# Attention, mixture of experts and a second feed-forward in one kernel: GpSimd work between scatters, other iterations for the first weights, the last attention iteration reordered

## The reference

```python
# 1. attention, B=4, H=8, S=576, D=64, causal window of 64
scores = where(0 <= row - col < 64, (q @ k.T) / sqrt(D), -1e9)
x = (softmax(scores) @ v)                 # -> [2304, 512]
# 2. mixture of 8 experts, two of them per token
noisy = x @ w_gate + log1p(exp(x @ w_noise)) * noise
top2, top2_w = the two largest of noisy, softmax of the two
out[token] += top2_w * (relu(x[token] @ w1[e]) @ w2[e])      # F = 1024
# 3. feed-forward
h = out @ w_in;  y = (h * clip(h + 3, 0, 6) / 6) @ w_out      # F2 = 2048
```

## Time and profile before

| | before |
|---|---|
| median of 3 runs | 1040.16 us (1039.94 to 1040.4) |
| profiled execution | 1048.24 us, its span 1046.5 us |
| PE busy / PEld busy | 96% / 85% of the span |
| DVE / ACT / POOL busy | 40% / 22% / 40% |
| first matmul of expert 0 (L1502) | starts at 158.16 us |
| PE busy before 160 us / after | 132.5 of 160 us / 876.5 of 886.5 us |

### The profile page before, as it was taken

One profiled execution on the slowest core, in us unless ns is written; L12 is line 12 of the kernel. 1 busy time (PEld: TensorE's weight loads), 2 busy tenths in 40 slices (PEclk: granted clock), 3 DMA queues, 4 the chain that ended last, 5 costly groups with the idle time before them and its releaser, 6 DMA issues.

```text
span 1046.5 us, 19876 instructions
## 1 busy us (share of the span) xinstructions
PE 1009.0 (96%) x8098; PEld 892.9 (85%) x8098; DVE 414.5 (40%) x879; ACT 234.0 (22%) x537; POOL 417.9 (40%) x276
## 2 busy tenths in 40 slices
PE   6899879999999999999999998999999999999998
PEld 5777658898999898999989987899999999999997
DVE  3466644322223122222222147644545445354433
ACT  4655531111111121111111112121111121111211
POOL 3555543898391918466482937400101001000000
PEclk9989879999999999999999999999999999999999
DMA  9877575867162625436251444110101001100000
GB/s 201 182 195 197 167 231 183 250 207 231 61 202 72 199 93 156 156 101 211 80 156 58 133 129 161 41 45 28 41 30 34 26 30 40 51 1 1 31 1 30
DMA packets 106793, 116.23 MB, mean 111 GB/s; under 512 B 27616, under 2 KB 74208, under 8 KB 106720
## 3 DMA queue, kind: packets, MB, share of 16 engines
q1 hardware_dynamic: 88672, 75.36, 25.6%
q10 hardware_dynamic: 12288, 20.98, 5.7%
q0 software_dynamic: 5760, 18.88, 5.4%
HBM read 76.13 MB, written 39.06 MB: 110 GB/s over the span
## 4 chain that ended last, share of the span: by engine, by line
PE 93%; DVE 3%; issue 1%; ACT 1%; DMA 1%; another core or an unknown queue 1%; ACTq 0%; DVEq 0%
PE PS L1502 21%; PE PS L1518 21%; PE PS L1629 18%; PE PS L1613 18%; PE PS L1307 2%; PE PS L1366 2%; PE PS L1387 2%; PE PS L1486 2%; PE PS L1350 2%; PE PS L1563 1%; PE PS L1399 1%; PE PS L1410 1%; PE PS L1328 1%; PE PS L1419 1%
## 5 line engine op out<-in xcount | busy, mean ns | idle before, releaser
L1518 PE MATMUL PS<-W,hs_room 128*128 128x512 f32 x960 | 245.8, 399 | 0.0
L1502 PE MATMUL PS<-xs,W 128*128 128x256 f32 (+1 forms) x1536 | 243.6, 309 | 1.1 <-issue 1.1
L1502 PEld LDWEIGHTS PS<-xs,W 128*128 128x128 f32 x1536 | 234.1, 189 | 11.7 <-issue 1.7
L1629 PE MATMUL PS<-W,gs 128*128 128x512 f32 x864 | 217.2, 396 | 3.3 <-DVE gs L1240 3.3
L1613 PE MATMUL PS<-x2s,W 128*128 128x384 f32 x1152 | 216.7, 337 | 0.6 <-issue 0.6
L1613 PEld LDWEIGHTS PS<-x2s,W 128*128 128x128 f32 x1152 | 201.3, 188 | 8.1 <-issue 1.0
L1518 PEld LDWEIGHTS PS<-W,hs_room 128*128 128x128 f32 x960 | 174.7, 188 | 33.7 <-issue 0.6
L641 POOL TENSOR_TENSOR W<-stage,ones_f 128x1024 fp32r<-128x1024 f32 x76 | 145.7, 1917 | 142.3 <-PE PS L1518 138.6
L1629 PEld LDWEIGHTS PS<-W,gs 128*128 128x128 f32 x864 | 161.3, 188 | 34.7 <-issue 4.6
L643 POOL TENSOR_TENSOR W<-stage,W 128x1024 fp32r<-128x1024 f32 x76 | 182.8, 2405 | 6.0
L1100 DVE SCALAR_TENSOR_TENSOR hs_room<-PS,hs_room 128x256 fp32r<-128x256 f32 (+1 forms) x128 | 62.8, 491 | 296.2 <-ACT hs_room L818 293.8
(11 more groups left out here) (132 smaller groups left out, 586.7 us busy)
## 6 DMA issues: line engine op xcount, KB each, us to landing
stage<-in_moe_w_dram SPq DMA_DIRECT2D x64, 512.0 KB
y_sorted<-y_sb ACTq DMA_DIRECT2D x40, 256.0 KB, 3.0
x_in<-x_sorted ACTq DMA_DIRECT2D x38, 256.0 KB, 4.9
x_sorted<-zeros SPq DMA_DIRECT2D x7, 1280.0 KB, 7.8
vD<-in_v_dram SPq DMA_DIRECT2D x72, 64.0 KB
out_dram<-o_sb SPq DMA_DIRECT2D x18, 256.0 KB, 2.1
stage<-in_moe_w_in_dram SPq DMA_DIRECT2D x8, 512.0 KB
stage<-in_moe_w_out_dram SPq DMA_DIRECT2D x8, 512.0 KB
```

The source lines that it names most:

```text
L1502: last = nc.tensor.matmul(HP_[:, c % 2, 0:n], W[:, par, 0, b, at:at + P], xs[part][:, a, kd, :], start=start, stop=(kd == KD - 1 and (a, b ...
L1518: last = nc.tensor.matmul(Y[:, first + t, :], hs[:, c % 2, a, t * P:(t + 1) * P], W[:, par, 1, b, c * DM:(c + 1) * DM], start=(c == 0 and ...
L1629: last = nc.tensor.matmul(OP[:, tt, :], gs[:, c % 2, a, tt * P:(tt + 1) * P], W[:, 1, c // FC, b, at:at + DM], start=(c == 0 and (a, b) == ...
```

## The change

On GpSimd no two scatters of lots 0 to 2 follow each other directly any more. In between stands the high part of a weight split, a `keep_x`, or a `pause`, a copy of 128x512 numbers into a buffer that nobody reads. The tables `FIRST_AT` and `SPLIT_AT` move loads and splits of the first weights to other iterations. The scatters of lot 2 (tiles 7 to 10) follow in one row after iteration 15, with `keep_x` of tiles 14, 15 and 16 among them. Of the zeros of `y_sorted`, two pieces stay in attention (iterations 15 and 16) and two go behind the first three x blocks and the four w1 chunks of expert 1. Iteration 18 is taken apart: its product with v comes first, and its gate and counting steps stand between the turns of the first x blocks.

```diff
-    FIRST_AT = (2, 3, 4, 5, 7, 8, 10, 11)
-    SPLIT_AT = (3, 4, 5, 6, 8, 9, 12, 13)
-    ZERO_AT = (14, 15, 16, 17)
+    FIRST_AT = (2, 4, 6, 8, 8, 10, 12, 12)
+    SPLIT_AT = (4, 6, 8, 9, 10, 12, 13, 14)
+    ZERO_AT = (15, 16)
+    ZERO_PARTS = 4
+    SCATTER_AT = {8: 0, 9: 1, 10: 2, 12: 3, 13: 4, 14: 5, 15: 6}
...
@@ SP
+            for n in range(len(ZERO_AT), ZERO_PARTS):
+                zero_y(n)
             sp.wait_ge(pads_ready, 1)
@@ GpSimd
+            def pause():
+                pool.wait_ge(paused, pauses[0])
+                pauses[0] += 1
+                nc.gpsimd.tensor_copy(idle[:], x_cur[:, 0]).then_inc(paused, 1)
+            for T in range(2, max(SCATTER_AT) + 1):
                 keep_x(T - 2)
-                now, later = SCATTER_AT.get(T, ((), ()))
-                for t, k in now:
-                    scatter(t, k)
-                if T in SPLIT_AT:
-                    split_first(SPLIT_AT.index(T))
-                if later:
-                    pool.wait_ge(sc_full, min(T + 2, TILES))
-                for t, k in later:
-                    scatter(t, k)
-            keep_x(TILES - 2)
+                if T in SCATTER_AT:
+                    scatter(SCATTER_AT[T], 0)
+                if T in SPLIT_AT:
+                    first_there(SPLIT_AT.index(T))
+                    split_hi(0, SPLIT_AT.index(T))
+                elif T in SCATTER_AT:
+                    pause()
+                if T in SCATTER_AT:
+                    scatter(SCATTER_AT[T], 1)
+                if T in SPLIT_AT:
+                    split_lo(0, SPLIT_AT.index(T), SPLIT_AT.index(T) + 1)
+            t0 = LOTS[FIRST_LOT][0]
+            for t in range(t0, t0 + LOTS[FIRST_LOT][1]):
+                for k in range(2):
+                    scatter(t, k)
+                    if t < t0 + 3 and k == 1:
+                        keep_x(max(SCATTER_AT) - 1 + t - t0)
+                    else:
+                        pause()
             keep_x(TILES - 1)
@@ DVE
-            for T in range(TILES + 1):
+            for T in range(TILES):
...
-            move_lg(TILES - 2)
+            move_lg(TILES - 3)
+            normalise(TILES - 1)
...
-            for j in range(PARTS[0][1]):
-                x_lo(0, j, Y[:, j, :])
+            x_lo(0, 0, Y[:, 0, :])
+            move_ga(TILES - 2)
+            x_lo(0, 1, Y[:, 1, :])
+            move_lg(TILES - 2)
+            x_lo(0, 2, Y[:, 2, :])
+            route(NB - 2, 5)
+            route(NB - 2, 6)
+            route(NB - 2, 7)
             move_ga(TILES - 1)
@@ TensorE
-            for T in range(LOOP[1], TILES + 1):
+            for T in range(LOOP[1], TILES):
                 iteration(T)
...
+                        if first and part == 0 and c == 1:
+                            rank_taken(NB - 2)
...
-            for j in range(PARTS[0][1]):
-                turn_x(0, j, Y[:, j, :])
+            times_v(TILES - 1)
+            gate_sum(TILES - 3)
+            transpose_x(TILES - 2)
+            turn_x(0, 0, Y[:, 0, :])
+            rank(NB - 2, TILES)
+            turn_x(0, 1, Y[:, 1, :])
+            gate_parts(TILES - 2)
+            turn_x(0, 2, Y[:, 2, :])
             gate_sum(TILES - 2)
             transpose_x(TILES - 1)
```

More of the change, by code:

```diff
@@ L129, in attention_moe_ffn @@
     xT = over("xT", [P, KD, P])
+    idle = over("idle", [P, DM])
     masks_in = over("masks_in", [P, (LOOP[1] - LOOP[0]) // LOOP_TILES, LOOP_TILES, P], BF16)
@@ L475, in zero_y @@
             def zero_y(n):
-                a, b = (FEWEST + (MOST - FEWEST) * m // len(ZERO_AT) for m in (n, n + 1))
+                a, b = (FEWEST + (MOST - FEWEST) * m // ZERO_PARTS for m in (n, n + 1))
                 sp.dma_start(y_sorted[a * P:b * P, :].rearrange("(p j) (k d) -> p (j k) d", p=P, d=P),
@@ L508, in _ @@
                     sp.dma_start(noise_sb[:], noise.rearrange("(t p) e -> p t e", p=P)).then_inc(s_small, 16)
-                if T in FIRST_AT:
-                    load_first(FIRST_AT.index(T))
+                for c in range(SCH):
+                    if FIRST_AT[c] == T:
+                        load_first(c)
                 if T == 6:
@@ L635, in _, with chunk_at, split_hi, split_lo @@
                         nc.gpsimd.tensor_copy(masks_in[part, (T - LOOP[0]) // LOOP_TILES, (T - LOOP[0]) % LOOP_TILES], masks[part, 2 * s + 1]).then_inc(m_all, 1)
-            def split(parity, c, n, halves):
[L638 to L643, removed]
+            def chunk_at(parity, c, a):
+                return W[:, parity, c // QCH, a, (c % QCH) * CH:(c % QCH + 1) * CH]
+            def split_hi(parity, c):
+                nc.gpsimd.tensor_tensor(chunk_at(parity, c, 0), stage[:, c % STAGES, :], ones_f[:].broadcast_to([P, CH]),
+                                        ALU.mult).then_inc(w_half, 1)
+            def split_lo(parity, c, halves):
+                pool.wait_ge(w_half, halves)
+                nc.gpsimd.tensor_tensor(chunk_at(parity, c, 1), stage[:, c % STAGES, :], chunk_at(parity, c, 0).bitcast(F32),
+                                        ALU.subtract).then_inc(w_ready, 1)
+            def split(parity, c, n, halves):
+                split_hi(parity, c)
+                split_lo(parity, c, halves)
             def split_set(m, parity):
@@ L672, in split_first @@
                     pool.wait_ge(ld_full, 4)
[L673 to L686 removed]
+            pauses = [0]
+            def pause():
[3 more added lines that the diff above has]
+            for T in range(2, max(SCATTER_AT) + 1):
+                keep_x(T - 2)
+                if T in SCATTER_AT:
[12 more added lines that the diff above has]
+                for k in range(2):
+                    scatter(t, k)
+                    if t < t0 + 3 and k == 1:
+                        keep_x(max(SCATTER_AT) - 1 + t - t0)
+                    else:
+                        pause()
             keep_x(TILES - 1)
@@ L797, in _ @@
                     move_pt(T, 0)
-                if 2 <= T <= TILES + 1:
+                if T >= 2:
                     move_xt(T - 2)
```

17 lines of the change are left out of this document (7 added, 10 removed).

## The result

| | before | after |
|---|---|---|
| median of 4 runs, us | 1040.05 (1039.65 to 1040.4) | 1047.74 (1046.88 to 1049.01) |
| ratio, 95% interval | | 1.0075 [1.0058, 1.0093] |
| profiled execution / span, us | 1048.24 / 1046.5 | 1046.88 / 1045.0 |
| first matmul of expert 0, us | 158.16 | 158.34 |

The change makes the kernel 0.75% slower, where 0.5% faster was forecast. The two profiles don't show this: the profiled execution of before took 8 us more than its other runs, that of after about its median. So first compare what happens inside them, and then ask what a usual execution of before looks like (the first experiment).

A forecast was written before the change was run, and what follows sets the result against it. Bound: TensorE's idle time before expert 0's first matmul at 158.16 us, from stalls taken as late instructions. Gains of 4.4 (chain) and 3.0 (early stalls) less 1.5 (clock) make 5.9 us: 1040.16 to 1034.3, said as 1034.5; range 1028 to 1044.

The forecast's parts named there:

- GpSimd in iterations 12 to 15: GpSimd's scatters, copies and moved splits there: no cost to TensorE while x_new's four buffers don't fill; iteration 15 ends at 125.1.
- Early stalls: Moving stage loads to other iterations shortens TensorE's stalls in 35-40, 50-55 and 85-90: 3.0 us gained, from -2 to 7.4.
- The base: Profiled execution lies 8.1 us above the runs' median; that difference was carried over, so 5.9 us came off 1040.16.
- Lot 2 and the chain: Scatters of lot 2 to expert 0: lot 2 starts at 129.6, first matmul at 153.8 for 158.16, 4.4 us gained.
- The landing of 4.5 us: Lot 1's scatter landing beside one piece of zeros, 4.5 us for 5.95, lets lot 2 begin at 129.6.
- 13.4 and 10.8 us: Lot 2's eight scatters, 13.4 us; then landing, x loads and the way from first turn to the expert's first matmul.
- The x wait and its clock price: TensorE idles before the first turn, about 140 to 148; the expert's first matmuls then cost 1.5 us more, between 0 and 3.
- The order itself: Reordered last iteration, tile 17's product with v ahead of counting: gains nothing, only places counting in an idle stretch.
- Late zeros: Two pieces of zeros behind weight chunks, with lot 3 later, after expert 0 starts: cost 0, bound 3 us.
- The slower rival: Stalls at 115 to 141 stay, so lot 2's scatters wait for tile 16: 1045 to 1046 us, chance 0.20.

The follow-up runs named there:

- the first experiment: The kernel before, unchanged, run and profiled again (also called e0): ratio to before 1.0006.
- e1: The changed kernel with the old FIRST_AT and SPLIT_AT tables: ratio to before 0.9995.
- e2: The kernel before with the new FIRST_AT and SPLIT_AT tables alone: ratio to before 1.0065.
- j3: The kernel before with stage loads of chunks 0 to 3 in iteration 1 and chunks 4 to 7 cut to 64 numbers a row: ratio to before 1.0002.
- e0: The kernel before, unchanged, run and profiled again: ratio to before 1.0006, on a chip where before takes 1037.79 us.
- h1: The changed kernel with the old tables and iteration 18 back in its old order: ratio to before 0.9998.
- h2: The kernel before with two of the four pieces of zeros moved behind the first x blocks: ratio to before 0.9991.
- e3: The changed kernel with splits moved off iterations 10 and 14, and some loads moved with them: ratio to before 1.0097.
- k4: The kernel before with all four pieces of zeros behind the first x blocks, repeated on another chip: ratio to before 0.9965.
- h3: The kernel before with all four pieces of zeros behind the first x blocks: ratio to before 0.9958.

## Why the prediction was wrong

- **The failed step** is the sentence on GpSimd in iterations 12 to 15 and on the tables, "The moved splits cost TensorE nothing as long as x_new's four buffers don't fill". GpSimd's own work was counted rightly, and the buffers didn't fill. What its operations do to DVE was not asked: the term was put at nothing. The runs showed that splits beside the choosing of experts stop DVE's small operations (3.08 us for one of 0.19) and that TensorE then waits for DVE (2.85 and 3.21 us); the two iterations grew by 4.9 and 3.5 us, 8.4 us in all, against e1, and the tables alone cost 0.65% (e2).
- **"Early stalls" 3.0 us**: 50-55 still has 2.94 us busy, 35-40 has 3.89 for 3.52, and in 85-90 the wait for DVE took the stall's place. In j3, without stage loads there, one gap stayed and one was halved, and the time didn't move. Nothing came of the term.
- **The base.** The working carried the 8.1 us between the profiled execution and the median over as a constant. Against e0 they lay mostly in the very stalls that the change was to remove, at 85 to 90, at 115 to 119 and in tile 15's product: the first two cost 4.8 us, and the third 3.1 (x_new from tile 14 to 15 takes 12.15 us in before, 9.03 in e0). Gains read from stalls that the timed runs don't have are not there to take.
- **Lot 2 and the chain, 4.4 us.** The landing of 4.5 us that was to set lot 2's start didn't: its rows did, at 131.13 and not 129.6. By the prediction's own links from there, 13.4 and 10.8 us, the expert's first matmul would come at 155.3. It came at 158.34: the eight scatters took 17.5 us for 13.4, since GpSimd waited 1.98 us for tile 15 and 2.13 us for tile 16, which was not in time; the 10.8 us behind them took 9.7.
- **The x wait and its clock price**: 5.36 us of idle, first matmuls 3.54 us against 3.56 in the earlier trace rows: the 1.5 us more were not paid in the first group, and in e1, behind a wait of 5.45 us, that group took 2.32 us. The order itself at 0 fits h1. Late zeros at 0 fit h2, where two were late; that all four late are a gain was missed.
- **The slower rival** had another mechanism, scatters that wait for tile 16. GpSimd does wait for it, 2.13 us, but the loss was made 20 to 50 us earlier. That this rival's time (1045 to 1046) lies near the measured one is luck.

## What to carry to other kernels

Before moving GpSimd work to another time, list what DVE does there: here operations of DVE between SBUF tiles were stopped until GpSimd's ended, and TensorE behind DVE paid, not GpSimd. When a profiled execution is slower than the median, find the place of the difference before predicting from it; here a second profile of the same kernel showed at once which stalls the timed runs don't have. And one chip's verdict on 0.7% can be none on the next: the change lost 0.75% in one set of runs and nothing in two others.

## What the runs showed of the hardware

- A DVE operation of about 0.2 us between SBUF tiles took up to 3.1 us beside a 128x1024 tensor_tensor of GpSimd: tensor_tensor (3.08), scalar_tensor_tensor (2.60 in e2), tensor_scalar (2.41), and a cast of 128x8 (2.52 in e3). x_new, with its large input in PSUM, kept its 0.69 us (e2, 83.61).
- TensorE's turns of k in iteration 9 came as 17 matmuls and drops of 4, 5 and 6 with 0.4 us of idle between, 3.1 us in place of 0.66, in the shown execution of before and alike in k4, and not in e0, the same program as before. Drops of other sizes stand in the profiles of all three slower chips.
- One program took 1038 to 1040 us in the median in two sets of runs and 1049 to 1050 us on three other chips.
- An indirect scatter's landing was waited for 6 to 8 us with zeros being written beside it; with none (h3, k4), lot 2 waited only 2.7 us, for DVE's rows.
